# A replanned instruction order, whole-tile copies and shorter GpSimd instructions in a chain of attention and two feed-forward networks

## The reference

```python
q_d, k_d, v_d = means of q, k, v over groups of 4 tokens      # 144 tokens
out_d = softmax(q_d @ k_d.T / 8) @ v_d                         # full attention on them
out_local = softmax(q @ k.T / 8 where |i - j| < 4) @ v         # band attention
x = repeat(out_d, 4) + out_local, heads side by side           # (4, 576, 512)
```

```python
u = x + real(fft(fft(x, axis=1), axis=2))
un = (u - mean(u)) / sqrt(var(u) + 1e-6)
x = u + relu(un @ w_ch1) @ w_ch2
h = relu(x @ w_in); c = conv3(h, conv_w)
out = (h * sigmoid(c)) @ w_out                                 # (4, 576, 512)
```

## Time and profile before

| | us |
|---|---|
| median of 3 runs | 880.51 |
| lowest and highest | 876.33, 881.18 |
| profiled execution, its time | 877.0 |
| its span | 875.1 |
| TensorE busy (7162 products) | 845.3 |
| VectorE busy | 454.6 |
| ScalarE busy | 309.0 |
| GpSimd busy | 251.1 |

### The profile page before, as it was taken

One profiled execution on the slowest core, in us unless ns is written; L12 is line 12 of the kernel. 1 busy time (PEld: TensorE's weight loads), 2 busy tenths in 40 slices (PEclk: granted clock), 3 DMA queues, 4 the chain that ended last, 5 costly groups with the idle time before them and its releaser, 6 DMA issues.

```text
span 875.1 us, 17508 instructions
## 1 busy us (share of the span) xinstructions
PE 845.3 (97%) x7162; PEld 787.1 (90%) x7162; DVE 454.6 (52%) x870; ACT 309.0 (35%) x942; POOL 251.1 (29%) x288
## 2 busy tenths in 40 slices
PE   8797999999999999999979999999999999999998
...
DMA packets 76617, 49.75 MB, mean 57 GB/s; under 512 B 60289, under 2 KB 65689, under 8 KB 76538
## 3 DMA queue, kind: packets, MB, share of 16 engines
...
## 4 chain that ended last, share of the span: by engine, by line
PE 86%; DVE 6%; SPq 2%; ACT 1%; DMA 1%; issue 1%; POOL 1%; DVEq 0%; ACTq 0%
PE banks L770 23%; PE banks L787 23%; PE banks L890 12%; PE banks L873 10%; PE banks L731 2%; PE banks L678 2%; PE banks L704 2%; PE banks L607 2%; PE banks L593 2%; PE banks L746 2%; PE banks L640 2%; PE banks L626 1%; PE banks L663 1%; PE banks L652 1%; PE banks L757 1%
## 5 line engine op out<-in xcount | busy, mean ns | idle before, releaser
L1238 DVE SCALAR_TENSOR_TENSOR hL<-banks,hH 128x256 fp32r<-128x256 f32 x144 | 60.8, 422 | 201.8 <-ACT hH L989 201.6
L989 ACT ACTIVATE hH<-banks 128x256 fp32r<-128x256 f32 x144 | 55.3, 384 | 263.9 <-PE banks L770 263.7
L1531 POOL TENSOR_TENSOR astage<-astage,rstd_bc 128x1024 f32<-128x1024 f32 x9 | 21.6, 2400 | 241.1 <-DVE astage L1367 241.1
L770 PE MATMUL banks<-unH,w1aH 128*128 128x256 f32 x288 | 86.2, 299 | 0.1
L787 PE MATMUL banks<-hH,w2aH 128*128 128x256 f32 x288 | 84.0, 292 | 0.0
L770 PE MATMUL banks<-unH,w1bH 128*128 128x256 f32 x288 | 82.4, 286 | 0.0
L770 PE MATMUL banks<-unL,w1aH 128*128 128x256 f32 x288 | 82.1, 285 | 0.0
L770 PE MATMUL banks<-unH,w1aL 128*128 128x256 f32 x288 | 82.1, 285 | 0.0
L770 PE MATMUL banks<-unH,w1bL 128*128 128x256 f32 x288 | 82.0, 285 | 0.0
L770 PE MATMUL banks<-unL,w1bH 128*128 128x256 f32 x288 | 82.0, 285 | 0.0
L787 PE MATMUL banks<-hH,w2bH 128*128 128x256 f32 x288 | 81.9, 284 | 0.0
...
## 6 DMA issues: line engine op xcount, KB each, us to landing
qk_in<-in_q SPq DMA_DIRECT2D x32, 144.0 KB, 2.6
qk_in<-in_k SPq DMA_DIRECT2D x32, 144.0 KB, 3.2
v_grp<-in_v SPq DMA_DIRECT2D x16, 288.0 KB
acc_dram<-astage SPq DMA_DIRECT2D x9, 512.0 KB, 3.3
astage<-acc_dram SPq DMA_DIRECT2D x9, 512.0 KB, 3.3
...
v_win<-in_v SPq DMA_DIRECT2D x32, 122.5 KB
w2araw<-in_moe_w_ch SPq DMA_DIRECT2D x4, 512.0 KB, 6.3
```

What stands on the lines that cost most here:

```text
L770: last = nc.tensor.matmul(bank[0][:, 0:CT], w[wp][:, t, P * m:P * m + P], (unH, unL)[xp][:, t, :], start=(t == 0 and i == 0), stop=(t == P ...
L989: nc.scalar.activation(hH[:, m % 2, :], bank[0][:, 0:CT], ACT.Relu).then_inc(hH_ok, 1)
L1238: nc.vector.scalar_tensor_tensor(hL[:, m % 2, :], bank[0][:, 0:CT], 0.0, hH[:, m % 2, :].bitcast(F32), ALU.max, ALU.subtract).then_inc(hL_ ...
L1531: nc.gpsimd.tensor_tensor(astage[:], astage[:], rstd_bc[:].unsqueeze(1).to_broadcast([P, PB, CT]), ALU.mult).then_inc(scaled, 1)
```

## The change

- **Order.** `PLAN` is a new list. In its first part all four quarters of w1 and three of w2 are loaded before q of pair 2; `wmeans.0.0` and the first two quarters of `centre_w1` and `round_w1` come before `flip_k.2`. It has 79 `warm` products where the old list has 60.
- **One copy each.** q and k of a pair are flipped and copied whole.
- **q's pooling** of pairs 0 to 3 goes from GpSimd (three additions) to VectorE (one reduction).
- **Small operations.** The 1e-9 of `invert` lies beside each row sum and is added by a reduction instead of a `tensor_scalar`; the maxima of the pooled scores go into PSUM, and their scaling reads them there.
- **GpSimd.** `low_w1` is four instructions of 128x256 instead of one of 128x1024; GpSimd's part of `fold_d` is done in halves of the tokens.
- **Table load.** ScalarE does one exponential of one column at its start.

```diff
-    load_q.0 load_k.0 load_c.0 load_w2.0.0 load_vg.0 warm.15 flip_q.0.0 load_w1.0.0 flip_q.0.1 keep_q.0.0 load_q.1
-    keep_q.0.1 pool_q.0 warm.2 flip_k.0.0 flip_k.0.1 keep_k.0.0 load_k.1 keep_k.0.1 pool_k.0 warm.2 score.0.0
-    score.0.1 mask.0.0 load_w1.0.1 top_l.0.0 score_d.0 pool_v.0 load_vw.0 mask.0.1 exp_l.0.0 top_l.0.1 top_d.0 warm.1
-    flip_q.1.0 exp_l.0.1 flip_q.1.1 invert.0.0 norm_l.0.0 load_q.2 exp_d.0 load_vg.1 keep_q.1.0 load_w2.0.1 invert.0.1
-    keep_q.1.1 warm.11 flip_k.1.0 norm_d.0 load_c.1 round_w2.0.0 flip_k.1.1 keep_k.1.0 keep_k.1.1 load_c.2 flip_p.0.0
-    norm_l.0.1 pool_k.1 score.1.0 pool_q.1 keep_p0.0 flip_p.0.1 score.1.1 mask.1.0 keep_p1.0 load_k.2 top_l.1.0
-    score_d.1 mask.1.1 exp_l.1.0 top_l.1.1 flip_pd.0 load_w1.0.2 top_d.1 pool_v.1 load_w1.0.3 keep_pd.0 invert.1.0
-    load_vw.1 low_w2.0.0 exp_d.1 warm.4 pooled.0 norm_l.1.0 flip_q.2.0 flip_q.2.1 keep_q.2.0 keep_q.2.1 keep_up.0
-    load_vg.2 pool_q.2 exp_l.1.1 warm.3 weigh.0.0 load_q.3 join.0.0 warm.1 weigh.0.1 load_w2.0.2 invert.1.1 join.0.1
-    norm_l.1.1 flip_k.2.0 load_vw.2 flip_k.2.1 keep_k.2.0 norm_d.1 keep_k.2.1 flip_p.1.0 pool_k.2 score.2.0 pool_v.2
-    keep_p0.1 flip_p.1.1 score_d.2 mask.2.0 keep_p1.1 load_k.3 top_l.2.0 flip_pd.1 top_d.2 exp_l.2.0 fold.0 load_vg.3
-    score.2.1 load_w2.0.3 exp_d.2 invert.2.0 mask.2.1 top_l.2.1 keep_pd.1 norm_l.2.0 exp_l.2.1 warm.9 flip_q.3.0
-    pooled.1 flip_q.3.1 load_q.4 keep_q.3.0 invert.2.1 keep_up.1 warm.1 flip_k.3.0 norm_l.2.1 keep_q.3.1 weigh.1.0
-    keep_k.3.0 flip_k.3.1 pool_q.3 join.1.0 flip_p.2.0 load_k.4 keep_k.3.1 weigh.1.1 keep_p0.2 norm_d.2 score.3.0
-    join.1.1 load_vw.3 pool_k.3 score.3.1 fold.1 mask.3.0 flip_p.2.1 top_l.3.0 score_d.3 keep_p1.2 mask.3.1 exp_l.3.0
-    top_l.3.1 flip_pd.2 top_d.3 flip_cw exp_l.3.1 keep_cw invert.3.0 warm.1 wmeans.0.0 norm_l.3.0 keep_pd.2 exp_d.3
-    flip_q.4.0 centre_w1.0.0 flip_q.4.1 pooled.2 load_q.5 keep_q.4.0 keep_q.4.1 invert.3.1 flip_k.4.0 keep_up.2
-    pool_q.4 flip_k.4.1 keep_k.4.0 round_w1.0.0 weigh.2.0 load_k.5 keep_k.4.1 flip_p.3.0 join.2.0 norm_l.3.1 score.4.0
-    pool_k.4 weigh.2.1 norm_d.3 mask.4.0 keep_p0.3 flip_p.3.1 load_vw.4 pool_v.3 score.4.1 top_l.4.0 keep_p1.3
-    join.2.1 exp_l.4.0 flip_pd.3 mask.4.1 centre_w1.0.1 score_d.4 fold.2 keep_pd.3 load_vg.4 invert.4.0 wmeans.0.1
-    top_d.4 round_w1.0.1 top_l.4.1 exp_d.4 norm_l.4.0 exp_l.4.1 fold_d.0.0 pooled.3 centre_w1.0.2 flip_q.5.0
-    flip_q.5.1 centre_w1.0.3 load_q.6 keep_up.3 keep_q.5.0 warm.1 weigh.3.0 keep_q.5.1 flip_k.5.0 round_w2.0.1
-    invert.4.1 flip_k.5.1 pool_q.5 load_k.6 join.3.0 keep_k.5.0 round_w2.0.2 warm.2 weigh.3.1 keep_k.5.1 norm_l.4.1
-    flip_p.4.0 join.3.1 load_vw.5 round_w1.0.2 score.5.0 norm_d.4 fold.3 flip_p.4.1 round_w1.0.3 low_w1.0.0 score.5.1
-    keep_p1.4 fold_d.0.1 round_w2.0.3 low_w1.0.1 mask.5.0 warm.7 feat.0.0.0 mask.5.1 top_l.5.0 feat.0.0.1 keep_cos.0.0
...
-    expand.8.6 contract.8.5 relu.8.6 split.8.6 expand.8.7 round_u.9.0 round_u.9.1 low_u.9.0 round_u.9.2 low_u.9.1
-    contract.8.6 round_u.9.3 low_u.9.2 relu.8.7 low_u.9.3 split.8.7 means.3.0 means.3.1 centre.3.0 expand.9.0
-    centre.3.1 contract.8.7 relu.9.0 split.9.0 square.3 keep_acc.8 store_acc.8 sum.3.1 vars.3 var_eps root rstd
-    flip_rstd keep_rstd store_rstd
+    load_q.0 load_k.0 load_vg.0 load_c.0 load_vw.0 warm.8 flip_q.0 keep_q.0 load_q.1 pool_q.0 load_vw.1 warm.4
+    flip_k.0 keep_k.0 pool_k.0 warm.3 score.0.0 pool_v.0 load_k.1 score_d.0 mask.0.0 load_c.1 score.0.1 top_d.0
+    load_w1.0.0 load_vg.1 top_l.0.0 exp_d.0 load_w1.0.1 mask.0.1 load_w2.0.0 top_l.0.1 exp_l.0.0 load_w2.0.1
+    load_w1.0.2 load_w1.0.3 exp_l.0.1 invert.0.0 load_w2.0.2 warm.11 flip_q.1 norm_l.0.0 load_q.2 keep_q.1 invert.0.1
+    load_w2.0.3 norm_l.0.1 load_c.2 pool_q.1 norm_d.0 warm.14 flip_k.1 keep_k.1 load_k.2 pool_k.1 warm.3 flip_p.0.0
+    flip_p.0.1 keep_p0.0 score.1.0 keep_p1.0 mask.1.0 pool_v.1 flip_pd.0 top_l.1.0 score_d.1 keep_pd.0 exp_l.1.0
+    top_d.1 pooled.0 load_vg.2 score.1.1 exp_d.1 invert.1.0 flip_q.2 mask.1.1 norm_l.1.0 load_q.3 flip_cw top_l.1.1
+    keep_up.0 keep_q.2 keep_cw weigh.0.0 exp_l.1.1 wmeans.0.0 join.0.0 pool_q.2 round_w2.0.0 invert.1.1 norm_l.1.1
+    low_w2.0.0 weigh.0.1 norm_d.1 load_vw.2 join.0.1 round_w2.0.1 centre_w1.0.0 fold.0 centre_w1.0.1 round_w1.0.0
+    warm.10 flip_k.2 load_k.3 keep_k.2 round_w1.0.1 pool_k.2 warm.3 flip_p.1.0 low_w1.0.0 flip_p.1.1 keep_p0.1
+    score.2.0 keep_p1.1 mask.2.0 flip_pd.1 top_l.2.0 low_w2.0.1 score.2.1 keep_pd.1 pool_v.2 exp_l.2.0 flip_q.3
+    pooled.1 mask.2.1 load_q.4 score_d.2 keep_q.3 invert.2.0 keep_up.1 pool_q.3 round_w2.0.2 weigh.1.0 norm_l.2.0
+    load_vg.3 wmeans.0.1 join.1.0 low_w1.0.1 top_l.2.1 top_d.2 exp_l.2.1 low_w2.0.2 weigh.1.1 exp_d.2 join.1.1
+    load_vw.3 warm.1 flip_k.3 fold.1 invert.2.1 keep_k.3 round_w2.0.3 pool_k.3 warm.3 score.3.0 load_k.4 mask.3.0
+    score_d.3 top_l.3.0 score.3.1 exp_l.3.0 top_d.3 norm_l.2.1 flip_p.2.0 norm_d.2 flip_p.2.1 keep_p0.2 keep_p1.2
+    pool_v.3 invert.3.0 mask.3.1 exp_d.3 warm.2 flip_pd.2 top_l.3.1 centre_w1.0.2 keep_pd.2 norm_l.3.0 load_vg.4
+    exp_l.3.1 warm.3 pooled.2 low_w2.0.3 flip_q.4 load_q.5 keep_up.2 invert.3.1 keep_q.4 warm.2 weigh.2.0
+    centre_w1.0.3 norm_d.3 round_w1.0.2 flip_k.4 pool_q.4 load_k.5 join.2.0 round_w1.0.3 keep_k.4 warm.2 weigh.2.1
+    pool_k.4 flip_p.3.0 load_vw.4 norm_l.3.1 score.4.0 join.2.1 low_w1.0.2 flip_p.3.1 mask.4.0 score_d.4 keep_p0.3
+    keep_p1.3 flip_pd.3 top_d.4 score.4.1 keep_pd.3 top_l.4.0 fold.2 mask.4.1 exp_d.4 flip_q.5 top_l.4.1 load_q.6
+    keep_q.5 warm.1 pooled.3 flip_k.5 keep_up.3 exp_l.4.0 weigh.3.0 keep_k.5 load_k.6 fold_d.0.0 join.3.0 score.5.0
+    exp_l.4.1 invert.4.0 weigh.3.1 pool_k.5 score.5.1 load_vw.5 join.3.1 fold.3 norm_l.4.0 pool_q.5 warm.5 flip_p.4.0
+    fold_d.0.1 pool_v.4 warm.4 score_d.5 top_d.5 feat.0.0.0 mask.5.0 exp_d.5 feat.0.0.1 keep_cos.0.0 low_w1.0.3
+    load_vg.5 mask.5.1 feat.0.1.0 keep_sin.0.0 invert.4.1 keep_p0.4 feat.0.1.1 keep_cos.0.1 top_l.5.0 feat.0.2.0
+    keep_sin.0.1 top_l.5.1 norm_d.4 exp_l.5.0 feat.0.2.1 keep_cos.0.2 norm_l.4.1 seq.0.0.0 pool_v.5 keep_sin.0.2
+    invert.5.0 exp_l.5.1 seq.0.0.1 flip_p.4.1 norm_l.5.0 load_vg.6 keep_qs.0.0 seq.0.1.0 keep_p1.4 turn.0.0 mix.0.0
+    flip_pd.4 turn.0.1 keep_pd.4 invert.5.1 seq.0.1.1 norm_l.5.1 seq.0.2.0 keep_qs.0.1 norm_d.5 mix.0.1 pooled.4
+    flip_q.6 keep_up.4 pool_v.6 weigh.4.0 keep_q.6 load_q.7 seq.0.2.1 join.4.0 seq.0.3.0 keep_qs.0.2 pool_q.6
+    load_vg.7 mix.0.2 flip_k.6 keep_k.6 load_k.7 seq.0.3.1 mix_p.0.2 pool_k.6 weigh.4.1 keep_qs.0.3 mix.0.3 flip_p.5.0
+    load_vw.6 flip_p.5.1 join.4.1 score.6.0 mix_p.0.3 keep_p1.5 keep_p0.5 score_d.6 mask.6.0 flip_pd.5 top_d.6 fold.4
+    round_u.0.0 round_u.0.1 score.6.1 low_u.0.0 round_u.0.2 exp_d.6 mask.6.1 low_u.0.1 keep_pd.5 low_u.0.2 round_u.0.3
+    top_l.6.0 pooled.5 low_u.0.3 flip_q.7 keep_up.5 pool_v.7 top_l.6.1 weigh.5.0 keep_q.7 load_q.8 expand.0.0 join.5.0
...
+    contract.8.2 relu.8.3 split.8.3 square.2 expand.8.4 contract.8.3 relu.8.4 split.8.4 sum.2.1 expand.8.5
+    contract.8.4 relu.8.5 split.8.5 expand.8.6 vars.2 relu.8.6 split.8.6 contract.8.5 sum.3.0 expand.8.7 round_u.9.0
+    round_u.9.1 low_u.9.0 round_u.9.2 low_u.9.1 means.3.0 relu.8.7 low_u.9.2 round_u.9.3 means.3.1 split.8.7 low_u.9.3
+    contract.8.6 centre.3.0 expand.9.0 centre.3.1 contract.8.7 square.3 keep_acc.8 relu.9.0 split.9.0 store_acc.8
+    sum.3.1 vars.3 var_eps root rstd flip_rstd keep_rstd store_rstd
...
-top_dn = [sb(f"top_d{u}", [P, NG3]) for u in range(2)]
...
-sums, sums_e, rsum = ([sb(f"{n}{u}", [P, NL + NG3]) for u in range(2)] for n in ("sums", "sums_e", "rsum"))
...
+sums = [sb(f"sums{u}", [P, NL + NG3, 2]) for u in range(2)]
+sums_e, rsum = ([sb(f"{n}{u}", [P, NL + NG3]) for u in range(2)] for n in ("sums_e", "rsum"))
...
+def halves(which):
+    return qkT[:, which, :].rearrange("p (g k) -> p g k", g=2)
...
+def pooled_tops(n):
+    return (bank[0] if n < PB else X)[:, 480:480 + NG3]
...
     def load_q(n):
-        at_least(sp, q_flipped, 2 * n)
+        at_least(sp, q_flipped, n)
...
     def load_k(n):
-        at_least(sp, k_flipped, 2 * n)
+        at_least(sp, k_flipped, n)
...
-    def flip_q(n, g):
-        if n == 0 and g == 0:
+    def flip_q(n):
+        if n == 0:
...
-            pe.wait_ge(k_kept, g + 1)
+            pe.wait_ge(k_kept, 1)
...
-        flip_half(0, g).then_inc(q_flipped, 1)
...
-    def flip_k(n, g):
+        flip_tiles(0).then_inc(q_flipped, 1)
...
+    def flip_k(n):
...
-        pe.wait_ge(q_kept, 2 * n + g + 1)
-        flip_half(1, g).then_inc(k_flipped, 1)
...
-    def flip_half(which, g):
-        for j in range(HT):
-            tile = qk_in[:, which, HT * g + j].rearrange("p two d -> p (two d)")
+        pe.wait_ge(q_kept, n + 1)
+        flip_tiles(1).then_inc(k_flipped, 1)
...
+    def flip_tiles(which):
+        for t in range(NT):
+            g, j = divmod(t, HT)
```

(88 more changed lines are left out.)

190 lines of the change are left out of this document (88 added, 102 removed).

## The result

| | us |
|---|---|
| median of 9 runs after, lowest and highest | 873.21 (870.4 to 874.62) |
| median of 9 runs before, beside them | 880.51 (876.33 to 881.88) |
| ratio, 95% interval | 0.9917 (0.9898 to 0.9937) |
| profiled execution after, its span | 874.62, 872.5 |

The change gains 0.8%, 7.3 us by the medians; 874.3 and a ratio of 0.993 were forecast. The profiled execution of after is the slowest of its nine, that of before (877.0) near the fastest, so the two traces differ by 2.4 us only (2.6 in their spans). The changed kernel ran again among the experiments: 871.3, with a span of 868.8 in its trace.

A forecast was written before the change was run, and what follows sets the result against it. TensorE was taken as the bound, with only the 118 us front and a little near 460 movable. Front -4.6, copies +0.5 and tail -2.1 make -6.2 us: 874.3 on the median, ratio 0.993, range 865 to 886.

The forecast's parts named there:

- The order of service: Front transfers: one queue in issue order at 234 KB/us, so q.2 lands at 31.2 us and k.2 at 38.7.
- The clock behind the wait: TensorE from `flip_q.2` to `flip_k.2`: a low clock after the wait for q.2 adds 3 us (bounds 0 and 4.1).
- the prices: TensorE steps priced by distance of starts in the stretch from 55.96 us, where it doesn't wait; sums multiplied by 0.925.
- Up to the first `feat`: TensorE from `flip_k.2`: 36.6 us of steps, 2 of fold wait, 1 of small waits; `feat` at 81.6 against 81.90.
- the step on the fold: Pair 3's fold on VectorE: wait before `feat` 2 us (bounds 0.1 and 6), was 6.28; short instructions' help not sure.
- From `feat` to `expand`: First `feat` to first `expand`: 31.7 us less 4.0 (bounds 0 and 6) taken back of 7.7 lost; `expand.0.0` at 109.3.
- Whole-tile copies: One copy each of q and k: VectorE saves 0.1 us, k flips wait; 0.5 us lost, 1 at most.
- new waits between 110 and 420: Sign of being wrong: new TensorE waits between 110 and 420 us, where attention is now denser.
- The tail: Near 420 to 462 us: TensorE's waits for sums of squares and rstd partly covered; 2.1 us gained (bounds 0 and 5).
- Costed at nothing: Early `pool_q`, table load and seven fewer warms are covered, worth nothing; pooled maxima and sums as reductions 0.1 us either way.
- all waits are met: Rival, 17%: q.2 at 26 us, clock stays up, fold hides; 12 us gained in front, 866 with the tail.
- the weights before q.2 make it slower: Rival, 20%: at `flip_q.2`, q.2 lands at 34.2 us; 886 in all; decided if `flip_k.2` starts later than about 46.

The follow-up runs named there:

- q2_first: Changed kernel with q of pair 2 loaded right behind k of pair 1, before all weights; 870.58 us, ratio 0.9893 to the kernel before.
- pairs_first: Changed kernel with only its front transfers reordered, q and k of pairs 2 and 3 ahead of weights needed later; 864.44 us, ratio 0.9822 to before.
- warm_in_wait: Changed kernel with 34 more products of the constant before the flip of q.2; 868.15 us, ratio 0.9862 to the kernel before.
- low_whole: Changed kernel with each `low_w1` one GpSimd instruction over 128x1024 again, `fold_d` still in halves; 878.0 us, ratio 0.9978 to the kernel before.
- tail_warm: Changed kernel with 12 products of the constant before `vars.3` and 6 before `flip_rstd`; 869.95 us, ratio 0.9899 to the kernel before.

## Why the prediction was right, and where not

**The order of service.** q.2 was forecast at 31.2 us and came at 32.09 and 30.88; `flip_k.2` at 41.9, and started at 43.27 and 42.48, with k.2 there; q2_first, where it waited for k.2, has it at 37.59, where 38.7 was forecast. Counting what is issued ahead by one rate was enough. The wait was 8 to 9 us instead of 5 to 6, since TensorE was done at 23.1, not 25 to 26: it costs nothing, as the end of the wait is set by the transfer. q2_first shows that it is the bytes, pairs_first that another order needs no wait.

**The clock behind the wait.** +3 was taken: from `flip_q.2` to `flip_k.2` it is 11.18 us against 7.7 by the prices, +3.5; warm_in_wait gets 3.2 of it back.

**Up to the first `feat`.** 36.6 of steps and 3 of waits from `flip_k.2` make 39.6, and 39.76 was measured (36.2 busy, 3.6 idle). The mechanism was the right one, `low_w1` away from the fold, but I gave its split forms too little: in the step on the fold short GpSimd instructions were "not sure" to help, and low_whole shows them to be worth 5 to 6 us of the 7.3 by the medians in this order, of which its trace ties 4.6 to the fold.

**From `feat` to `expand`.** 27.7 was forecast (31.7 - 4.0), 25.10 measured: 6.6 of the 7.7 us lost come back, more than the bound of 6. The low clock before is gone here altogether; what is left is 1.17 us of waiting before one `pooled`. That no low clock follows this wait is partly luck of the execution: it did in five of the traces above. `expand.0.0` is at 108.13, 5.8 better than the old kernel's 113.95 at the same sum of steps, where 4.6 was forecast.

**Whole-tile copies.** 0.5 us lost was forecast. Four flips wait for a whole copy of q, 0.8 us in all in after's table of waits, but between 108 and 415 us TensorE is idle for 3.0, where it was 0.7: 1.8 of it is the wait at `wmeans.1.0`, which no step of the prediction has, though it named new waits between 110 and 420 as a way to be wrong. The new list issues the second half of w1 at 319.74 us (331.84 before) and asks for it 5.5 us behind that, in front of the `feat` steps; before, these stood in between and it was asked for after 9 us. Its four transfers take 4.2 to 7.6 us to land. No run has the copies halved again, so their own price is not shown.

**The tail: this step failed.** Forecast were 2.1 us: "`contract.8.6` stands behind `means.3` and covers 1.4", `relu.9.0` takes back 0.8, the two other waits give 1.2 and the clock the rest. The chain that ended last in before, from `means.3.1` on, and then that in after (pieces of issue under 0.05 us are left out):

```profile
448.73 0.50 PE banks L801 x2
449.25 2.63 DVE cent L1268 x2
451.90 2.13 ACT cent L993
454.06 1.37 DVE part L1259
455.45 0.77 DVE total L1263
456.26 1.38 PE banks L807 x12
```

```profile
443.12 1.14 DVE unL L1239 x3
444.27 0.34 DVE hL L1244
444.61 0.33 DVE unL L1239
444.94 2.54 DVE cent L1274 x2
447.50 2.13 ACT cent L992
449.63 0.28 ACT hH L988
449.93 0.04 DVE hL L1244
449.97 0.30 issue
450.27 1.36 DVE part L1265
451.65 0.77 DVE total L1269
452.47 2.09 PE banks L807 x12
```

From the first product of `means.3.1` (448.56 and 443.56) to the end of the wait it was 7.70 us and is now 8.91. `contract.8.6` does cover 1.4, but 1.2 of it are lost again: 0.6 because `centre` on VectorE now stands behind `low_u.9` and `split.8.7` when `means.3.1` is there, which no step of the prediction has, and 0.6 because VectorE's `split.9.0` waits for `relu.9.0` behind the square, which was priced at 0.8. So the last wait is 3.46 instead of 3.70. Of the two other waits the one of 0.36 is gone and the one of 0.82 is as before: 0.4 us gained, not 1.2. The clock was the largest miss. It is low for 10.2 us in both traces of the changed kernel, where it was for 6.9 in the one trace of before. From `means.3.1` to the end of the third step behind `flip_rstd`, `contract.8.6` left out, after takes 18.3 us and before 17.4: 1 us worse, not 2.1 better. tail_warm, which fills these waits, takes 3.3 us off this stretch.

**The sum.** -5.8 us for the front, +2.3 behind it and +1.0 in the tail are -2.5, and the spans differ by 2.6. The forecast of -6.2 fits the medians (-7.3) better than this pair of traces, and partly by luck, because errors cancel: the front gave more, the rest less. Which of the terms the fast executions of before lack is open, as only one trace of it was read.

**Costed at nothing.** The small operations, the table load, `pool_q` on VectorE and seven `warm` fewer were covered as said.

**Rivals.** That all waits are met (866) was refused by q.2 at 31 to 32; that the weights before q.2 make it slower decides at 46 us for `flip_k.2`, and that came at 43.3. But the place was rightly named: pairs_first took 6.9 us from there.
